# Second expert layer: relu rows transposed within their own step, weight conversions by half chunks, nested loop conditions, the last tile in two column halves

## What is computed

```python
logits = x @ w_gate + modality_bias[modality_id]        # x: 1536 x 512
e_idx = np.argmax(logits, axis=1)
gate_w = softmax(logits)[np.arange(N), e_idx]
for e in range(E):                                      # E = 8
    mask = e_idx == e
    h = np.maximum(x[mask] @ w1[e], 0.0)                # w1[e]: 512 x 1024
    out[mask] = gate_w[mask, None] * (h @ w2[e])        # w2[e]: 1024 x 512
```

## Time and profile before

| | |
|---|---|
| median of 3 runs | 666.13 us (665.6 to 666.72) |
| profiled execution, its own time | 671.87 us |
| its span in the trace | 669.7 us |
| TensorE matmul busy | 640.5 us, 96%, 3866 matmuls |
| VectorE busy | 330.2 us, 49% |
| ScalarE busy | 276.2 us, 41% |
| GpSimd busy | 185.5 us, 28% |
| matmuls of the second layer, per line | L1342 x112, L1373 x112 (8 per tile, 14 tiles) |
| conversions of the second layer's later experts | L1458 x8, L1829 x8 (two experts) |

### The profile page before, as it was taken

How to read it: one execution, slowest core, us unless ns; L and a number is a source line. 1 busy time by engine, 2 the same in 40 slices (tenths; PEclk the granted TensorE clock), 3 DMA queues, 4 the chain that set the end, 5 groups by cost and what they waited for, 6 DMA issues and landing times.

```text
span 669.7 us, 11241 instructions
## 1 busy us (share of the span) xinstructions
PE 640.5 (96%) x3866; PEld 581.3 (87%) x3867; DVE 330.2 (49%) x681; ACT 276.2 (41%) x529; POOL 185.5 (28%) x199
## 2 busy tenths in 40 slices
PE   7989999897999999999999999999988999999994
PEld 6989999896999999999999999997866888788883
DVE  4466645585654625437163452557786422452221
ACT  5667866541343525344252423232634321441220
POOL 2501100116435351614416150300553111211201
PEclk9999999998999999999999999999899999999998
DMA  7867822173566664636556340351828710110100
GB/s 208 284 213 243 296 91 80 65 252 73 177 158 191 157 184 140 151 105 133 184 144 179 117 89 3 49 187 37 270 54 309 289 34 32 36 32 32 47 16 27
DMA packets 51089, 89.84 MB, mean 134 GB/s; under 512 B 7919, under 2 KB 14063, under 8 KB 51040
## 3 DMA queue, kind: packets, MB, share of 16 engines
q1 hardware_dynamic: 41872, 69.21, 30.9%
q0 software_dynamic: 9168, 19.97, 13.5%
HBM read 73.13 MB, written 17.02 MB: 135 GB/s over the span
## 4 chain that ended last, share of the span: by engine, by line
PE 82%; DVE 8%; issue 3%; ACT 3%; DMA 2%; SPq 1%; ACTq 0%; DVEq 0%; POOL 0%; POOLq 0%
PE banks L1060 6%; PE banks L1059 6%; PE banks L1078 6%; PE banks L999 6%; PE banks L1001 6%; PE banks L998 6%; PE banks L803 4%; PE banks L831 4%; PE banks L1342 4%; PE banks L1377 3%; PE banks L1343 3%; PE banks L1347 3%; PE banks L1373 3%; PE banks L1374 3%; PE banks L815 2%
## 5 line engine op out<-in xcount | busy, mean ns | idle before, releaser
L1833 DVE TENSOR_TENSOR split<-stage,split 128x2048 fp32r<-128x2048 f32 x32 | 73.3, 2291 | 41.8 <-ACT split L1463 41.7
L998 PE MATMUL banks<-xTs,split 128*128 128x416 f32 (+1 forms) x256 | 88.6, 351 | 0.0
L999 PE MATMUL banks<-xTs,split 128*128 128x416 f32 (+1 forms) x256 | 86.4, 342 | 0.0
L650 POOL DMA_INDIRECT x_moe<-rows,dst_idx x25 | 49.3, 1971 | 113.0 <-DVE rows L2285 112.1
L1059 PE MATMUL banks<-hTs,split 128*128 128x416 f32 x224 | 79.9, 357 | 0.0
L1060 PE MATMUL banks<-hTs,split 128*128 128x416 f32 x224 | 78.6, 351 | 0.0
L1598 ACT ACTIVATE hTs<-banks 128x416 fp32r<-128x416 f32 x56 | 29.0, 518 | 81.6 <-PE banks L1001 81.6
L1463 ACT ACTIVATE split<-stage 128x2048 fp32r<-128x2048 f32 x32 | 61.0, 1908 | 1.2 <-DMA stage<-w1a 1.2
L1720 ACT ACTIVATE hTs<-banks 128x512 fp32r<-128x512 f32 x28 | 16.5, 596 | 104.2 <-PE banks L1357 104.2
L1001 PE MATMUL banks<-xTs,split 128*128 128x416 f32 (+1 forms) x256 | 56.2, 341 | 0.0
L803 PE MATMUL banks<-k_sb,q_sb 128*128 128x260 f32 (+2 forms) x192 | 49.9, 386 | 3.4 <-DMA k_sb<-k_w 1.9
(11 more groups left out here) (371 smaller groups left out, 1312.1 us busy)
## 6 DMA issues: line engine op xcount, KB each, us to landing
stage<-w1a SPq DMA_DIRECT2D x16, 1024.0 KB
stage<-w2a SPq DMA_DIRECT2D x16, 1024.0 KB, 5.6
k_sb<-k_w SPq DMA_DIRECT2D x12, 520.0 KB, 5.1
raw<-w1b SPq DMA_DIRECT2D x4, 1024.0 KB
raw<-w2b SPq DMA_DIRECT2D x4, 1024.0 KB, 10.6
q_sb<-q_t SPq DMA_DIRECT2D x24, 128.0 KB, 3.1
x_attention<-rows SPq DMA_DIRECT2D x12, 256.0 KB, 5.8
split<-x_moe SPq DMA_DIRECT2D x12, 256.0 KB, 3.7
```

What stands on the lines that cost most here:

```text
L650: pool.indirect_dma_start(out=x_dram[1], out_offset=rows_at(dst_idx[0], early_dst, e, k), in_=y_lines(e, k), in_offset=None, compute_op=AL ...
L998: pe.matmul(psum, piece(slot, 0, o + c * FH), xTs[:, 0, c, 0:cols], start=(c == 0), stop=False)
L999: pe.matmul(psum, piece(slot, 1, o + c * FH), xTs[:, 0, c, 0:cols], start=False, stop=False)
L1833: dve.tensor_tensor(split_chunk(e % 2, 1, c), staged_chunk(e % 2, c), split_chunk(e % 2, 0, c).bitcast(F32), ALU.subtract).then_inc(low_do ...
```

## The change

1. **Turning in the own step.** `second(t-1)` now takes the tile whose relu rows are to be turned: after its first half comes th(t, 0), after its second half th(t, 1). A step is first(t, 0), first(t, 1), tx(t+1), then second(t-1) with the two in it. On ScalarE `h_high(t, ...)` stands at the end of step t, behind `next_weights`; on VectorE h_low(t, 0) stands behind `next_weights`, then the row copy, then h_low(t, 1).
2. **Half chunks.** A conversion of 2048 columns becomes two of 1024 on both engines; VectorE starts on a half when ScalarE has finished it. TensorE still waits for whole chunks.
3. **Nested conditions.** The condition of the second tile of an iteration, and GpSimd's for gathers, stand inside that of the first. TensorE reads the number of tiles ahead of its first loop.
4. **The last tile.** Its 24 second matmuls of 512 columns become 48 of 256: all of the left half, then all of the right, each in a bank of its own (6 and 7). VectorE copies each half when it is done; the scatter waits for both.

The diff, cut to its core:

```diff
+PIECE = CHUNK // 2
...
+        psEnd = [banks[:, 6 + side, 0:D // 2] for side in range(2)]
...
             with pool.Fori(LEAST2 // 2 - 1, (MOE2_TILES + 1) // 2) as r:
-                for b in range(2):
-                    with pool.If(r * 2 + (b + 3) < tiles):
-                        gather(r * 2 + (b + 3), 1 - b)
-                    with pool.If(r * 2 + b < tiles):
-                        scatter(r * 2 + b, b, r)
+                with pool.If(r * 2 < tiles):
+                    with pool.If(r * 2 + 3 < tiles):
+                        gather(r * 2 + 3, 1)
+                    scatter(r * 2, 0, r)
+                    with pool.If(r * 2 + 1 < tiles):
+                        with pool.If(r * 2 + 4 < tiles):
+                            gather(r * 2 + 4, 0)
+                        scatter(r * 2 + 1, 1, r)
...
-                def second(t, e, slot):
+                def second(t, e, slot, turned=None):
...
-                    mm.then_inc(y_done, 1)
+                        if half == 1:
+                            mm.then_inc(y_done, 1)
+                        if turned is not None:
+                            th(turned, half)
+
+                def last_second(e, slot):
+                    for side in range(2):
+                        for c in range(FC):
+                            if side == 0 and c % 4 == 0:
+                                pe.wait_ge(low_done[2 + c // 4], e + (E + 1))
+                                pe.wait_ge(h_high_done, end * 2 + (c // 4 + 1))
+                            o = DC * F + c * D + side * D // 2
+                            for part in range(2):
+                                pe.matmul(psEnd[side], hTs2[:, 0, c, :], half_weights(slot, part, o), start=(c == 0 and part == 0), stop=False)
+                        for c in range(FC):
+                            if side == 0 and c % 4 == 0:
+                                pe.wait_ge(h_low_done, end * 2 + (c // 4 + 1))
+                            mm = pe.matmul(psEnd[side], hTs2[:, 1, c, :], half_weights(slot, 0, DC * F + c * D + side * D // 2),
+                                           start=False, stop=(c == FC - 1))
+                        mm.then_inc(y_done, 1)
...
                     first(t, 0, e, slot)
-                    th(t - 1, 0)
                     first(t, 1, e, slot)
-                    th(t - 1, 1)
...
-                    second(t - 1, before_e, before_slot)
+                    second(t - 1, before_e, before_slot, t)
...
-                second(2, e2, slot2)
+                second(2, e2, slot2, 3)
...
                 with pe.Fori(sure // 2 - 1, (NT + 1) // 2) as r:
                     with pe.If(r * 2 < tiles):
                         step(r * 2, 0, r + 1, tiles)
-                    with pe.If(r * 2 + 1 < tiles):
-                        step(r * 2 + 1, 1, r + 2, tiles)
-                th(end, 0)
-                th(end, 1)
-                second(end, e, slot)
+                        with pe.If(r * 2 + 1 < tiles):
+                            step(r * 2 + 1, 1, r + 2, tiles)
+                last_second(e, slot)
...
-                act.activation(split[:, bass.ds((n + 1) % 2 if slot is None else slot, 1), 0, c * CHUNK:(c + 1) * CHUNK].rearrange("p a n -> p (a n)"),
-                               raw[:, c, :], ACT.Copy).then_inc(high_done[c], 1)
+                at = bass.ds((n + 1) % 2 if slot is None else slot, 1)
+                for piece in range(2):
+                    o = c * CHUNK + piece * PIECE
+                    act.activation(split[:, at, 0, o:o + PIECE].rearrange("p a n -> p (a n)"),
+                                   raw[:, c, piece * PIECE:(piece + 1) * PIECE], ACT.Copy).then_inc(high_done[c], 1)
...
                     act.wait_ge(th_done, t * 2 + (half + 1))
-                    act.wait_ge(y_done, t + 1)
+                    if half == 1:
+                        act.wait_ge(y_done, t + 1)
...
                 def step(t, tiles=None):
-                    h_high(t - 1, 0)
+                    if isinstance(t, int):
+                        h_high(t - 1, 0)
                     relu(t, 0)
-                    h_high(t - 1, 1)
+                    if isinstance(t, int):
+                        h_high(t - 1, 1)
                     relu(t, 1)
...
                     next_weights(t)
+                    h_high(t, 0)
+                    h_high(t, 1)
...
+                def last_y_copy(b):
+
+                    for side in range(2):
+                        at = slice(side * D // 2, (side + 1) * D // 2)
+                        dve.wait_ge(y_done, end + (2 + side))
+                        if side == 0:
+                            dve.wait_ge(scattered[b], went * 16)
+                        copied = dve.tensor_scalar(y_sb[:, b, at], psEnd[side], slot_gate[:, bass.ds(end, 1)], None, ALU.mult)
+                    copied.then_inc(y_copied, 1)
...
-                        gated(dve, "dve", high_done[c], e + (E + 2))
-                        low_part(None, c, slot)
+                        gated(dve, "dve", high_done[c], e * 2 + (E + 2))
+                        low_piece(c, 0, slot)
+                        gated(dve, "dve", high_done[c], e * 2 + (E + 3))
+                        low_piece(c, 1, slot).then_inc(low_done[c], 1)
...
                     next_weights(t)
+                    h_low(t, 0)
                     y_copy(t - 1, 1 - b, went)
+                    h_low(t, 1)
```

More of the change, by code:

```diff
@@ L1331, in weights, with half_weights @@
                     return split[:, bass.ds(slot, 1), part, o:o + 512].rearrange("p a n -> p (a n)")
+                def half_weights(slot, part, o):
+                    return split[:, bass.ds(slot, 1), part, o:o + D // 2].rearrange("p a n -> p (a n)")
                 def first(t, half, e, slot):
@@ L1431, in second_layer @@
                 tx(4, 0, 3)
-                second(2, e2, slot2)
-                with pe.Fori(2, sure // 2 - 1) as r:
-                    step(r * 2, 0, r + 1)
-                    step(r * 2 + 1, 1, r + 2)
+                second(2, e2, slot2, 3)
                 more = pe.value_load(used[0:1, 1, 0:1], min_val=0, max_val=NT - sure)
@@ L1439, in second_layer @@
                 e, slot = expert(end)
+                with pe.Fori(2, sure // 2 - 1) as r:
+                    step(r * 2, 0, r + 1)
+                    step(r * 2 + 1, 1, r + 2)
                 with pe.Fori(sure // 2 - 1, (NT + 1) // 2) as r:
@@ L1794, in expert_phase @@
                 next_weights(2)
-                with act.Fori(3, sure - 1) as t:
+                step(3)
+                with act.Fori(4, sure - 1) as t:
                     step(t)
@@ L1798, in expert_phase @@
                 tiles = act.snap(more + sure)
-                end = act.snap(more + (sure - 1))
                 with act.Fori(sure - 1, NT) as t:
@@ L1802, in expert_phase @@
                         step(t, tiles)
-                h_high(end, 0)
-                h_high(end, 1)
             first_layer()
@@ L1823, in link, with low_piece @@
                 dve.wait_ge(chain, links[0])
[L1825 to L1829 removed]
+            def low_piece(c, piece, slot):
+                at, o = bass.ds(slot, 1), c * CHUNK + piece * PIECE
+                hi, lo = (split[:, at, k, o:o + PIECE].rearrange("p a n -> p (a n)") for k in range(2))
+                return dve.tensor_tensor(lo, raw[:, c, piece * PIECE:(piece + 1) * PIECE], hi.bitcast(F32), ALU.subtract)
             def first_layer_low(e, c):
@@ L2457, in step @@
                 def step(t, b, went, tiles=None):
[L2458 to L2459 removed]
+                    if isinstance(t, int):
+                        h_low(t - 1, 0)
+                        h_low(t - 1, 1)
                     if tiles is None:
@@ L2516, in expert_phase @@
                         step(r * 2, 0, r - 1, tiles)
-                    with dve.If(r * 2 + 1 < tiles):
-                        step(r * 2 + 1, 1, r, tiles)
-                h_low(end, 0)
-                h_low(end, 1)
+                        with dve.If(r * 2 + 1 < tiles):
+                            step(r * 2 + 1, 1, r, tiles)
                 for b in range(2):
                     with dve.If(parity == b):
-                        y_copy(end, b, went)
+                        last_y_copy(b)
             first_layer()
```

10 lines of the change are left out of this document (3 added, 7 removed).

## The result

| | before | after |
|---|---|---|
| median | 666.27 us (665.56 to 671.24, 7 runs) | 661.13 us (659.23 to 663.98, 7 runs) |
| profiled execution, its own time | 671.87 us | 659.96 us |
| its span | 669.7 us | 657.7 us |

The ratio of the medians is 0.9923 with a 95% interval of 0.9902 to 0.9944: 5.1 us less, where -4.74 was forecast. The gain is clear of the noise, though small. The two profiled executions differ by 11.9 us. Of that, 6.8 us had come about before the transposes of x for the loops began (505.47 us from the start before, 498.69 after), in stages that the change does not touch. All that follows is therefore read from stretches inside the second layer.

The account below looks back on a forecast made before the run. TensorE hardly ever stands still in the second layer, so only its three idle places and the end behind its last product count. Terms sum to -4.74 us from the 666.13 us median: 661.4 us, 8-in-10 range 659.8 to 663.8.

Parts of the forecast that it names:

- Term 1: Expert change before tile 8: half chunks shorten the conversion chain, h's transposes lengthen its cover; -1.75 us.
- Rival A: Expert change: the wait before tile 8 stays wholly or half; 662.3 or 663.2 us, chance 0.12.
- Term 2: Wait before tile 2: relu stands behind two half conversions on ScalarE; +0.1 us (0 to 0.2).
- Term 3: TensorE's steps: three groups of transposes instead of two, one more switch per step; +0.25 us over some nine steps.
- Terms 4, 5 and 6: After the last step: less TensorE idle time -2.07 us, 256-column products +0.2, shorter last copy -0.27.
- the exit: TensorE's queue leaving the loop after the last step: 2.9 us over four empty iterations, hidden by 3.6 us of lead.
- The wait for the second high copy: Last tile's products: ScalarE's second copy takes 1.2 us against 0.94 of narrow products; 0.3 us stay idle.
- Term 7: GpSimd's way out after the last scatter: shorter walk, so the scatter's landing ends last; -1.2 us (0 to 1.6).
- Rival B: End of kernel: the scatter lands as late as GpSimd's loop ends, nothing gained there; 662.6 us, chance 0.13.
- Rival C: Steps: h's transposes at two new places break TensorE's stream, 11.7 us lost; slower, 673.1 us, chance 0.05.
- Rival D: Code fetch: conditions jumping over two steps cost 1 us more each, about 3.3 us lost; 664.7 us, chance 0.08.

Follow-up runs that it names:

- e12: e11 with TensorE's loads of the number of tiles and last expert moved from ahead of its first loop into tile 3's products; 660.44 us, ratio 0.9913.
- e7: Changed kernel with the surely empty iterations on TensorE and GpSimd passed over by one condition; 665.79 us, ratio 0.9923 to the kernel before.
- e5: Changed kernel with TensorE's two conditions of an iteration side by side again, GpSimd's still nested; 662.6 us, run once.
- e4: Changed kernel with h's transposes, high copies and low parts back one step later, all else kept; 667.74 us, ratio 0.9954 to the kernel before.
- e8: Changed kernel with all last-tile products ordered high and low of blocks 0 to 3, then of 4 to 7; 662.0 us, run once.
- e11: Changed kernel with the edits of e7 and e8 together; 660.25 us, ratio 0.9913 to the kernel before.
- e1: Changed kernel with GpSimd's conditions in its last loop side by side again; 666.45 us, ratio 0.9958 to the kernel before.
- e9: Changed kernel with e7's single condition and last-tile products 512 columns wide, in normal step order, own bank, one copy; 660.08 us, run once.

## Why the prediction was right

The sum came out within 0.5 us, by terms of which two were off and one was missing.

**Term 1 (-1.75)** measured -1.69. The two runs with one side each show both mechanisms at nearly the size given: 0.78 for the halves (0.9 forecast, though the chains of the sum, 7.2 and 6.4 us, differ by 0.8) and 0.87 for the transposes as cover. One step of the sum is miscounted without harm: 1024 columns at 0.88 ns are 0.90 us, not 0.86, so the sum gives 1.01 us for a half, not 1.05; four took 3.91 us. Rival A (the wait stays) is out: 0.10 us is left.

**Term 2 (+0.1)** is not shown as such. Tiles 2 to 4 took 0.09 us longer, and four half conversions take 3.91 us where two whole ones took 3.72, so 0.1 us per additional instruction. But the one step in question takes 8.94 to 9.30 us in the kernels with halves, and 9.05 and 8.91 in the two with whole chunks. The Trainium skill (VectorE: DVE Perf Modes, The TRN2 errata) gives ScalarE a fixed latency of 224 cycles per instruction that reads SBUF, by the page's 1.2 GHz an estimated 0.19 us. In these traces an additional conversion right behind another costs half of that, (3.91 - 3.72)/2 = 0.095 us.

**Term 3 (+0.25)**: 0.05 us per step, 12.34 against 12.29, so more than the 0.03 per group that was taken; over three steps +0.14. Four later ones show none, since before the change one of them held the 0.22 us of the load of the number of tiles, which moved. That load is the **missing term**: the prediction does not count TensorE's loads at their new place. Ahead of the first loop they meet a queue that has no lead, and with the last expert's number they cost 0.35 us, of which the chain of waits shows a slower start:

```profile
523.05 0.44 PE banks L1365 x4
523.49 0.12 issue
523.61 0.49 PE banks L1350
```

e12 confirms it by taking it away.

**Terms 4, 5 and 6 (-2.07 + 0.2 - 0.27 = -2.14)** measured -1.91 together. The step that was off is the exit: I took 3.6 us of lead and 2.9 us of way out, "so the exit is hidden". The queue's loop branches run from 643.4 to 646.5:

```profile
L1465 PEldq COMPARE_BRANCH  x5: 83/221/235, 643.4 to 646.5; - x5
```

The lead was there: at 643.4 TensorE still had work until 646.86, 3.5 us. The way out was longer than the term had it. The branches take 3.1 us, not 2.9, and from the last of them it is another 0.7 us to the first narrow product at 647.18, which the term left out. 3.8 less 3.5 us leave the 0.32 that are visible, and the late queue slows the first 16 narrow products to 0.149 us each; in e7 the 0.32 are gone and these 16 take 0.29 us less. (The expectation of e5 counts way and lead as 3.3 and 3.1 us; these do not give 0.32.) Both edits were needed: with turning alone 1.99 us stay idle (e5), with nesting alone 0.73 us on ScalarE's copy (e4).

The wait for the second high copy was put at 0.3 us and measures 0.13 (e8) and 0.17 (e11). Narrow products run at 0.120 us once the queue is in time, so 48 of them take 5.76 us, +0.3 against 5.46, not +0.2. The last copy saves 0.27 us as forecast, and some 0.25 us more because its address was worked out ahead: it starts 0.02 us after the last product, before the change 0.28.

**Term 7 (-1.2)** measured -2.2: the largest error. The mechanism was right. e1 gives back 2.16 us, and e7 shows that nothing more is to be had by a shorter walk, since the landing ends the span. But 2.2 us lie outside the term's own bounds of 0 to 1.6. The size failed at two steps. The first is "a gather lands 3.3 us after its issue, which for the scatter is 667.9": in the changed kernel the wait for the landing is over 2.6 us after the issue, 0.7 us sooner. The second stands unsaid in the sum: its 1.2 us are 669.1, the last semaphore instruction, less 667.9, which keeps the 0.6 us from there to the span's end. Where the landing ends the span, 0.3 us are left (657.4 to 657.7); why is open. Both together are the 1.0 us. Rival B is out.

**Rival C** (slower by broken streams) is out: 12.34 us per step. **Rival D** as well. The jump over both steps costs 0.215 us, and over one step 0.208 before. TensorE's queue, condition of the first tile (ns min/median/max, starts):

```profile
L1466 PEldq COMPARE_BRANCH  x4: 213/215/218, 643.8 to 646.1; - x4
```

The Trainium skill (Runtime: NRT & Kernel Launch, Instruction fetch mechanics) has a taken branch out of the window wait for its page; on this loop, passed four times in a row, no such wait is to be seen. Whether these jumps leave the window no row shows.

So the error of 1.0 us in term 7 was in part made good by the missing 0.35 us and the 0.2 us at the end. That the total fits within 0.5 us is partly luck, and it does not prove the terms.

## What to carry to other kernels

Ask of each engine's queue how far it is ahead where a loop ends, and how long it takes over the iterations that do nothing: conditions side by side instead of nested cost 1.7 us on TensorE (3.0 in the one execution, in which the clock fell as well) and 2.2 us on GpSimd here. The iterations could be seen in the queues' own rows. Count the way to the first product behind the loop as well. Loads that feed registers belong where the queue has a lead, not at the entry of a loop. And a wait that a conversion causes can be shortened from both sides, by smaller pieces and by work moved into its shadow; here the two added up.

## What was not expected of the hardware

**The clock falls after short idle times, in some executions.** Every kernel here has a gap at the same place, around tile 2's first transposes, while weights are converted. In the changed kernel it is 1.25 us, four transposes, and 0.66 us. In 12 of 14 profiled executions the granted clock stayed at 1.00 and this step took 8.9 to 9.3 us; in e7 it took 10.94 (clock 0.50 from 521 to 523 us), in e12 10.60. The windows of e12 (columns as above):

```profile
508.00:512.00 4.00, 2.64 (x15) 1.85 (x13) 2.96 (x3) 3.47 (x6) 0.94 (x2) 1.00 0.99 373
512.00:513.00 1.00, 0.62 (x3) 0.56 (x4) 0.69 (x1) 1.00 (x2) 1.00 (x2) 1.00 1.04 406
513.00:517.00 4.00, 4.00 (x12) 3.13 (x11) 3.40 (x3) 3.12 (x5) 0.04 (x1) 0.57 1.06 402
517.00:521.00 4.00, 4.00 (x23) 3.38 (x22) 2.12 (x4) 1.68 (x4) 0.00 (x0) 1.00 1.04 383
```

and of the changed kernel at the same place, with a gap slightly longer:

```profile
506.00:510.00 4.00, 2.58 (x15) 1.82 (x13) 3.00 (x3) 3.36 (x5) 1.01 (x2) 1.00 1.04 391
...
511.00:515.00 4.00, 4.00 (x19) 3.30 (x19) 3.51 (x4) 3.54 (x5) 0.16 (x1) 1.00 1.05 392
```

In e12 the granted clock fell towards 0.50 (1.2 GHz) once the products ran again, and came back to 1.00 (2.4 GHz) during them. Products behind the gap begin 0.43 us apart instead of 0.23 for some 4 us, and about 1.5 us are lost. That is more than the gain of any edit at the end of e11 or e12, and it may be part of why runs of one kernel differ by 2 to 4 us: of the seven runs of the result, the fastest (659.23 us) has a mean granted clock of 0.999, the slowest (663.98) one of 0.991. The totals alone do not show that the falls behind this gap make that difference. What decides whether the clock falls stays open; the gaps alone do not tell it (e12 had 1.08 and 0.66 us, less than the changed kernel; e7 had 1.94 and 0.33).

**A scatter ends sooner than a gather**: 2.8 us from issue to landing for 0.26 MB in the changed kernel (2.7 in e9, e11 and e12), against 3.3 us for the gather of the earlier trace rows. The last scatter moves 0.18 MB; by GpSimd's last semaphore instruction the wait for it ends after 2.6 us here and up to 3.0 us in e9.
